# Row-limited moves of the partly filled slot tile, and the last expert's closing matmuls in another order

## The chip, the cores and the metric

The kernel runs on one core of one Trainium2 chip. The metric is device microseconds of one execution. Five engines work side by side, each in the order of its own queue: TensorE (PE in the profile, with its weight loads as PEld), VectorE (DVE), ScalarE (ACT), GpSimd (POOL) and SyncE (SP, here only issuing transfers). They meet through semaphores.

## The reference, cut to what matters

Three layers follow each other. The change touches only the third.

```python
x = attention(q, k, v, centroids)            # 2 x 8 heads, 768 rows of 64, masked by cluster
x = gelu(x @ w_in) @ w_out                   # 1536 tokens, 512 -> 2048 -> 512
logits = x @ w_gate + log1p(exp(x @ w_noise)) * noise
top2 = two largest of the 8 experts; top2_w = softmax over these two
for e in range(8):
    out[mask] += top2_w * (relu(x[mask] @ w1[e]) @ w2[e])    # 512 -> 1024 -> 512
```

## The kernel before, in words

**Slots.** Each token is written, by indirect transfers on POOL's queue, to a slot of each of its two experts in the table slot_x in memory. An expert has CAP = 448 slots: YT = 4 tiles of 128 rows, of which the fourth (index FULL = 3) has only REST = 64 rows. Before an expert runs, SP loads its slots into slot_rows (128 x 4 x 512), and TensorE turns them, so that the 512 features lie on partitions. One pass c (of DC = 4) turns 128 features: four transposes, one for each tile, into one PSUM bank. ACT and DVE then split the bank's 448 columns into a high and a low part (sx_hi, sx_lo). The fourth transpose reads all 128 rows, though only 64 were loaded. POOL's memset in line 676 has set the other 64 rows to zero once, the semaphore rest_cleared says so, and TensorE waits for it (line 1035). All transposes are in transpose mode.

**The first expert** is special. When it should start, the last 512 tokens aren't routed yet. `route_last` therefore first turns the already stored rows (`kept_slots`, eight transposes, then the small matmuls of `ranks`, then eight more), and `move_rows` adds the last tokens' rows onto the same banks with matmuls against 0/1 matrices (`moves`, built by DVE line 1602 from the result of `ranks`). Eight idle matmuls (line 831) stand ahead of the first transposes.

**The other experts.** `turn_slots(n + 1, part)` turns the rows of the next expert in the middle of expert n: part 0 (two passes, eight transposes) behind the last up-projection, part 1 behind the down-projection of piece 6. This happens for n = 0 to 6, seven times.

**The MLP of an expert** has eight pieces of 128 hidden units: `up` makes a piece (12 matmuls, each product in three parts of the fp32r type), ACT (line 1311) and DVE (line 1745) apply relu and split it (hid_done counts that), and `down` adds it to the four output banks: three matmuls for each full tile, two for the fourth tile, since its 64 columns of high and low part lie side by side. The fourth tile comes second in the order in which the last expert is closed: ORDER = (0, 3, 1, 2).

**The end.** In the last expert `down_end` does the pieces 5, 6 and 7 tile by tile. Its list of steps runs

```python
steps = [(0, last_piece - 2), (0, last_piece - 1), (1, last_piece - 2), (1, last_piece - 1),
         (0, last_piece), (1, last_piece)]
```

so that two tiles' pieces 5 and 6 come ahead of the first wait for piece 7. Meanwhile POOL gathers the rows of the other experts (line 647, got and acc; line 695, slot_rows), DVE adds them (line 1785) and SP stores the tokens. After that DVE scales the last gathers (line 1796), adds the last expert's tiles to them (`take_end`, lines 1808 and 1817), and POOL writes each tile to the output with an indirect transfer (line 703).

Of the kernel before, what the change touches and what calls it, by code (L numbers as in the profile page):

```python
# [19 lines left out]
P = 128  # L20
# [14 lines left out]
FULL = CAP // P  # L35
REST = CAP - FULL * P
YT = FULL + 1
GROUP = 256
RING = 4
# [35 lines left out]
def clustered_attention_ffn_moe(nc, q, k, v, centroids, w_in, w_out, w_gate, w_noise, noise, w1, w2, out):  # L75
    B, H, D, S = q.shape
    C = centroids.shape[1]
    DM, FF = w_in.shape
    E, _, FE = w1.shape
    N = B * S  # L80
    J = S // P
# [10 lines left out]
    GP = GROUP // P  # L92
# [28 lines left out]
    with ctx:  # L121
        def sem(name):
            return ctx.enter_context(nc.semaphore(name))

        def alloc(where, name, shape, dt):
            return where.enter_context(nc.sbuf_tensor(name, shape, dt))

        psum = ctx.enter_context(nc.psum_tensor("psum", [P, 8, 512], F32))


        ident = alloc(ctx, "ident", [P, P], F32)
# [81 lines left out]
        slot_rows = alloc(ffn, "slot_rows", [P, YT, DM], F32)  # L213
# [73 lines left out]
        group_used = sem("group_used")  # L287
        hid_ready = sem("hid_ready")
        hid_act = sem("hid_act")
        hid_done = sem("hid_done")  # L290
# [18 lines left out]
        rounds_ready = sem("rounds_ready")  # L309
        sx_in = sem("sx_in")  # L310
        slot_of_set = sem("slot_of_set")
        rest_cleared = sem("rest_cleared")
        split_hi = sem("split_hi")
        split_lo = sem("split_lo")
        moves_ready = sem("moves_ready")
# [29 lines left out]
        ORDER = (0, FULL) + tuple(range(1, FULL))  # L345

        def rows_of(j):

            return P if j < FULL else REST
# [73 lines left out]
        def turn_bank(c, first):  # L423

            return 4 + c if first else 6 + c % 2
# [155 lines left out]
        def _(pool):  # L581
# [90 lines left out]
                scatter_chunk(t)  # L672
            chain.link(nc.gpsimd.iota(slot_i[:], pattern=[[1, CAP]], base=-FAR, channel_multiplier=0))
            nc.gpsimd.tensor_copy(slot_of[:], slot_i[:]).then_inc(slot_of_set, 1)
            pool.wait_ge(slot_of_set, 1)
            nc.gpsimd.memset(slot_rows[REST:P, FULL], 0.0).then_inc(rest_cleared, 1)
            pool.wait_ge(sx_in, 2 * DMA)
            scatter_chunk(CHUNKS - 1)

            for j in range(YT):  # L680
                first = LAST_SLOT + j * P
# [57 lines left out]
        def _(pe):  # L739
            mm = nc.tensor.matmul  # L740

            def bank(n):
                return psum[:, n]
# [84 lines left out]
            def idle_rows(count, at):  # L828

                for _ in range(count):  # L830
                    mm(bank(at), ident_b[:], zeros[:].bitcast(BF16)[:, 0:CT], start=True, stop=True)
# [75 lines left out]
            def down_tile(f, slot, rest, j, pieces, held=None):  # L907

                held = f % 2 if held is None else held
                dst = bank(j)  # L910
                if rest and j == FULL:

                    both = hid_hi[:, held, j * P:]
                    mm(dst, both, down_hi[:, slot, f % GP], start=(f == 0), stop=False)
                    return mm(dst, both, down_lo[:, slot, f % GP], start=False, stop=(f == pieces - 1))  # L915
                cols = slice(j * P, (j + 1) * P)
                mm(dst, hid_hi[:, held, cols], down_hi[:, slot, f % GP], start=(f == 0), stop=False)  # L917
                mm(dst, hid_hi[:, held, cols], down_lo[:, slot, f % GP], start=False, stop=False)  # L918
                return mm(dst, hid_lo[:, held, cols], down_hi[:, slot, f % GP], start=False, stop=(f == pieces - 1))  # L919
# [11 lines left out]

            def down_end(piece0, pieces):

                last_piece = pieces - 1
                steps = [(0, last_piece - 2), (0, last_piece - 1), (1, last_piece - 2), (1, last_piece - 1),
                         (0, last_piece), (1, last_piece)]
                steps += [(i, f) for i in range(2, YT) for f in range(last_piece - 2, pieces)]
                for i, f in steps:
                    if i == 0:
                        pe.wait_ge(hid_done, piece0 + f + 1)  # L940
                    last = down_tile(f, f // GP % RING, True, ORDER[i], pieces, 2 if f == last_piece else None)
                    if i == YT - 1 and f % GP == GP - 1:
                        last.then_inc(group_used, 1)
                    elif i < YT - 1 and f == last_piece:
                        last.then_inc(y_ready, 1)

            def layer(pieces, width, rest, piece0, group0, chunk, moving_hi, moving_lo, turn, after=None,
# [23 lines left out]
            def turn_rows(f, to):  # L971

                for c in range(DC):
                    last = nc.tensor.transpose(psum[:, to, c * P:(c + 1) * P], y_sb[:, f, c * P:(c + 1) * P], ident[:])
                last.then_inc(yt_ready, 1)
# [14 lines left out]
            def ranks(p, at):  # L990

                pe.wait_ge(sel_ready, p + 1)
                for j in range(TPC):
                    dst = psum[:, at, RANK0 + j * E:RANK0 + (j + 1) * E]
                    for i in range(j):
                        mm(dst, ones_b[:], r_sel[:, i], start=(i == 0), stop=False)
                    mm(dst, before[:], r_sel[:, j], start=(j == 0), stop=True)
                for i in range(TPC):
                    last = mm(psum[:, at, RANK0 + TPC * E:RANK0 + (TPC + 1) * E], ones_b[:], r_sel[:, i],
                              start=(i == 0), stop=(i == TPC - 1))  # L1000
                last.then_inc(rank_ready, 1)

            def logits(p, j, held, at):
                if j == 0:
                    pe.wait_ge(slots_ready, LEAD + p)
                pe.wait_ge((yt_act, yt_dve)[j % 2], 2 * p + j // 2 + 1)
                for c in range(DC):
                    last = mm(psum[:, at, j * 2 * E:(j + 1) * 2 * E], yt[:, held, c * P:(c + 1) * P], wr[:, c],
                              start=(c == 0), stop=(c == DC - 1))
                if j == TPC - 1:  # L1010
                    last.then_inc(logits_ready, 1)
# [14 lines left out]
            def route_last(p):  # L1026

                pe.wait_ge(slots_ready, LEAD + p)
                for f in range(TPC):
                    pe.wait_ge((y_act, y_dve)[f % 2], LEAD + 2 * p + f // 2 + 1)  # L1030
                    turn_rows(f, 4 + f)
                for f in range(TPC):
                    logits(p, f, f, LAST)
                pe.wait_ge(sx_in, 2 * DMA)
                pe.wait_ge(rest_cleared, 1)
                idle_rows(8, FULL)
                for c in range(DC // 2):
                    kept_slots(c)
                ranks(p, LAST)
                for c in range(DC // 2, DC):  # L1040
                    kept_slots(c)
                for c in range(DC):
                    move_rows(c)

            def kept_slots(c):

                for j in range(YT):
                    mm(psum[:, turn_bank(c, True), j * P:(j + 1) * P], slot_rows[:, j, c * P:(c + 1) * P], ident[:],
                       is_transpose=True, start=(j == 0), stop=False)

            def move_rows(c):

                dst = psum[:, turn_bank(c, True), 0:CAP]
                for j in range(TPC):
                    if c == 0:
                        pe.wait_ge(split_lo, j + 1)
                        pe.wait_ge(moves_ready, j + 1)
                    mm(dst, row_hi(j)[:, c * P:(c + 1) * P], moves(j), start=False, stop=False)
                    last = mm(dst, row_lo(j)[:, c * P:(c + 1) * P], moves(j), start=False, stop=(j == TPC - 1))
                last.then_inc(sx_turned, 1)  # L1060

            route_last(CHUNKS - 1)

            PIECE0 = CHUNKS * (FF // P)

            def turn_slots(n, part, first=False):

                if part == 0:
                    pe.wait_ge(sx_in, 2 * DMA * (n + 1))
                for c in (2 * part, 2 * part + 1):  # L1070
                    if not first:
                        pe.wait_ge(sx_done, n * DC + max(c - 1, 0))
                    for j in range(YT):
                        last = nc.tensor.transpose(psum[:, turn_bank(c, first), j * P:(j + 1) * P],
                                                   slot_rows[:, j, c * P:(c + 1) * P], ident[:])
                    last.then_inc(sx_turned, 1)

            def expert_step(n, last, end=False):
                layer(FE // P, CAP, True, PIECE0 + n * (FE // P), EXPERT0 + n * EGR, CHUNKS + n,
                      lambda c: sx_hi[:, c], lambda c: sx_lo[:, c],  # L1080
                      (lambda part: None) if last else (lambda part: turn_slots(n + 1, part)),
                      turned_in=n * DC, end=end)
# [812 lines left out]
```

## Time and profile before

| | us |
|---|---|
| three runs | 921.95, 918.08, 920.74 |
| median | 920.74 |
| profiled execution, its own time | 921.95 |
| its span, first to last instruction | 920.2 |
| TensorE busy (matmuls) in the span | 897.9 |
| DVE / ACT / POOL busy | 528.1 / 420.9 / 143.6 |
| mean granted TensorE clock, share of full | 0.984 |

The profiled execution took 1.75 us more than its span. In the page a matmul's end is modelled: consecutive matmuls overlap in it, so the distance from one start to the next is what a matmul costs in a row of many, not its duration. In views that merge a run of equal instructions, x8 stands for eight of them and the second number is the time of the run.

### The profile page before, as it was taken

How to read it: one execution, taken by the hardware profiler on the slowest of the kernel's cores; microseconds unless marked ns; L12 is line 12 of the kernel's file. 1: busy time of each engine (PE TensorE's matmuls, PEld its weight loads, DVE VectorE, ACT ScalarE, POOL GpSimd, SP SyncE). 2: the span in 40 equal slices, each digit the busy share in tenths (PEclk: the TensorE clock that was granted, in tenths of full speed). 3: DMA queues.
4: the chain of work that ended last, by engine and by line, in shares of the span. 5: the costliest groups of instructions: out<-in, count | busy, mean ns of one | idle time of the engine just before them, and what ended most of it. 6: DMA issues, size and time to landing. Idle time of an engine off the chain costs nothing.

```text
span 920.2 us, 12560 instructions
## 1 busy us (share of the span) xinstructions
PE 897.9 (98%) x4353; PEld 736.0 (80%) x4355; DVE 528.1 (57%) x959; ACT 420.9 (46%) x689; POOL 143.6 (16%) x147
## 2 busy tenths in 40 slices
PE   6999999999999999999999999999999999999995
PEld 4777777777776888888888888888888888888884
DVE  6688887887866444436443645644345343434383
ACT  4577767777668222344234323424434243433420
POOL 2021221221222000002300140500000000005073
PEclk8899999999999999999999999999999999999998
DMA  5123332331353323323532343625252544527464
GB/s 125 35 70 106 94 104 67 113 109 44 97 199 134 134 99 113 116 85 120 169 123 91 125 150 130 222 95 197 95 186 89 190 146 145 170 92 268 164 195 164
DMA packets 84302, 119.00 MB, mean 129 GB/s; under 512 B 19258, under 2 KB 47930, under 8 KB 84256
## 3 DMA queue, kind: packets, MB, share of 16 engines
q1 hardware_dynamic: 79328, 104.08, 35.1%
q0 software_dynamic: 4928, 14.35, 4.5%
q8 instruction: 24, 0.39, 0.2%
q14 instruction: 22, 0.18, 0.1%
HBM read 89.12 MB, written 29.39 MB: 129 GB/s over the span
## 4 chain that ended last, share of the span: by engine, by line
PE 78%; DVE 9%; issue 5%; POOL 4%; DMA 1%; ACT 1%; SPq 1%; POOLq 0%; DVEq 0%; ACTq 0%
PE psum L818 10%; PE psum L902 9%; PE psum L904 9%; PE psum L903 9%; PE psum L917 8%; PE psum L919 8%; PE psum L918 8%; PE psum L783 3%; PE psum L803 3%; PE psum L804 3%; DVE neg_max L1432 2%; POOL got L647 2%; POOL acc L647 1%; DVE recip L1456 1%; PE psum L915 1%
## 5 line engine op out<-in xcount | busy, mean ns | idle before, releaser
L818 PE MATMUL psum<-probs,vx 128*128 128x386 f32 x384 | 156.4, 489 | 0.4 <-ACT probs L1141 0.4
L917 PE MATMUL psum<-down_hi,hid_hi 128*128 128x512 f32 x384 | 151.1, 393 | 0.7 <-DVE hid_lo L1704 0.7
L919 PE MATMUL psum<-down_hi,hid_lo 128*128 128x512 f32 x384 | 149.9, 390 | 0.0
L918 PE MATMUL psum<-down_lo,hid_hi 128*128 128x512 f32 x384 | 149.9, 390 | 0.0
L1311 ACT ACTIVATE hid_hi<-psum 128x448 fp32r<-128x448 f32 x64 | 35.0, 546 | 180.4 <-PE psum L904 180.4
L1141 ACT ACTIVATE probs<-psum 128x384 f32<-128x384 f32 x192 | 90.5, 489 | 55.9 <-PE psum L804 53.3
L1432 DVE TENSOR_REDUCE neg_max<-psum 128x1 f32<-128x768 f32 x96 | 91.3, 955 | 25.8 <-PE psum L783 22.2
L1745 DVE SCALAR_TENSOR_TENSOR hid_lo<-psum,hid_hi 128x384 fp32r<-128x384 f32 x64 | 35.6, 556 | 117.4 <-ACT hid_hi L1311 117.4
L1284 ACT ACTIVATE gelu<-psum 128x512 f32<-128x512 f32 x48 | 28.7, 598 | 157.2 <-PE psum L904 157.2
L803 PE MATMUL psum<-qa,ka 102*128 102x384 f32 x192 | 93.9, 489 | 0.6 <-DVEq L1445 0.5
L903 PE MATMUL psum<-sx_lo,up_hi 128*128 128x448 f32 x256 | 93.5, 365 | 0.0
L902 PE MATMUL psum<-sx_hi,up_hi 128*128 128x448 f32 x256 | 93.5, 365 | 0.0
L904 PE MATMUL psum<-sx_hi,up_lo 128*128 128x448 f32 x256 | 93.5, 365 | 0.0
L1467 DVE TENSOR_TENSOR up_lo<-raw,up_hi 128x1024 fp32r<-128x1024 f32 x56 | 68.5, 1222 | 38.6 <-ACT down_hi L1176 38.5
L919 PEld LDWEIGHTS psum<-down_hi,hid_lo 128*128 128x128 f32 x384 | 72.0, 188 | 15.5
L917 PEld LDWEIGHTS psum<-down_hi,hid_hi 128*128 128x128 f32 x384 | 72.1, 188 | 14.7 <-issue 1.1
L918 PEld LDWEIGHTS psum<-down_lo,hid_hi 128*128 128x128 f32 x384 | 72.2, 188 | 13.9
L1703 DVE CAST hid_hi<-gelu 128x512 fp32r<-128x512 f32 x48 | 20.8, 432 | 106.5 <-ACT gelu L1284 106.5
L902 PE MATMUL psum<-xt_hi,up_hi 128*128 (+1 forms) x192 | 76.3, 398 | 0.0
L904 PE MATMUL psum<-xt_hi,up_lo 128*128 (+1 forms) x192 | 74.9, 390 | 0.0
L903 PE MATMUL psum<-xt_lo,up_hi 128*128 (+1 forms) x192 | 74.8, 389 | 0.0
L618 POOL TENSOR_TENSOR off<-less_sum,near 64x384 f32<-64x384 f32 x32 | 39.8, 1245 | 216.7 <-ACT near L1156 216.7
(208 smaller groups left out, 1548.1 us busy)
## 6 DMA issues: line engine op xcount, KB each, us to landing
raw<-in_moe_w SPq DMA_DIRECT2D x64, 512.0 KB, 4.2
raw<-in_moe_w_in SPq DMA_DIRECT2D x24, 512.0 KB, 3.5
raw<-in_moe_w_out SPq DMA_DIRECT2D x24, 512.0 KB, 5.1
slot_x<-zeros SPq DMA_DIRECT2D x7, 1024.0 KB, 5.6
slot_rows<-slot_x SPq DMA_DIRECT2D x8, 768.0 KB, 6.7
raw_q<-in_q SPq DMA_DIRECT2D x30, 192.0 KB, 3.3
raw_k<-in_k SPq DMA_DIRECT2D x30, 192.0 KB, 3.7
slot_y<-y_sb SPq DMA_DIRECT2D x7, 768.0 KB, 3.6
```

Source lines behind the costliest of these rows:

```text
L618: nc.gpsimd.tensor_tensor(off[rows], less_sum[rows], near[rows], ALU.mult).then_inc(off_ready, 1)
L803: mm(dst, ka[0:ROWS, n % SLOTS, keys], qa[0:ROWS, n % SLOTS, queries], start=True, stop=False)
L818: mm(psum[:, 5 + half, 0:WIDE], vx[:, n % 2, c], probs[:, at % SLOTS], start=(c == 0), stop=(c == J - 1)).then_inc(unit_done, 1)
L902: mm(dst, up_hi[:, slot, c, cols], moving_hi(c), start=(c == 0), stop=False)
L903: mm(dst, up_hi[:, slot, c, cols], moving_lo(c), start=False, stop=False)
L904: last = mm(dst, up_lo[:, slot, c, cols], moving_hi(c), start=False, stop=(c == DC - 1))
L917: mm(dst, hid_hi[:, held, cols], down_hi[:, slot, f % GP], start=(f == 0), stop=False)
L918: mm(dst, hid_hi[:, held, cols], down_lo[:, slot, f % GP], start=False, stop=False)
L919: return mm(dst, hid_lo[:, held, cols], down_hi[:, slot, f % GP], start=False, stop=(f == pieces - 1))
L1141: copy(probs[:, at % SLOTS, 0:HALF], psum[:, 2 + at % SLOTS, 0:HALF], ACT.Exp, scale=float(D) ** -0.5)\
L1432: dv.tensor_reduce(neg_max[:, m % 2, i:i + 1], psum[:, held:held + 2, 0:HALF], AX.XY, ALU.max, negate=True)\
L1467: dv.tensor_tensor(up_lo[:, slot], raw1[:, stage], up_hi[:, slot].bitcast(F32), ALU.subtract)
```

## The change

It does three things.

1. The fourth tile's transposes take only its 64 loaded rows, against a 64 x 64 identity, and write 64 columns. The memset, its semaphore and TensorE's wait are gone.
2. `kept_slots` no longer sets transpose mode: its 16 products are ordinary fp32 matmuls against the identity.
3. `down_end` closes one tile after another: all of pieces 5, 6, 7 of tile 0, then of the fourth tile, then of tiles 1 and 2.

```diff
-            pool.wait_ge(slot_of_set, 1)
-            nc.gpsimd.memset(slot_rows[REST:P, FULL], 0.0).then_inc(rest_cleared, 1)
...
-                last_piece = pieces - 1
-                steps = [(0, last_piece - 2), (0, last_piece - 1), (1, last_piece - 2), (1, last_piece - 1),
-                         (0, last_piece), (1, last_piece)]
-                steps += [(i, f) for i in range(2, YT) for f in range(last_piece - 2, pieces)]
-                for i, f in steps:
+                for i, j in enumerate(ORDER):
+                    for f in range(pieces - 3, pieces):
...
-                pe.wait_ge(rest_cleared, 1)
...
-                    mm(psum[:, turn_bank(c, True), j * P:(j + 1) * P], slot_rows[:, j, c * P:(c + 1) * P], ident[:],
-                       is_transpose=True, start=(j == 0), stop=False)
+                    rows = rows_of(j)
+                    mm(psum[:, turn_bank(c, True), j * P:j * P + rows], slot_rows[0:rows, j, c * P:(c + 1) * P],
+                       ident[0:rows, 0:rows], start=(j == 0), stop=False)
...
-                        last = nc.tensor.transpose(psum[:, turn_bank(c, first), j * P:(j + 1) * P],
-                                                   slot_rows[:, j, c * P:(c + 1) * P], ident[:])
+                        rows = P if j < FULL else REST
+                        last = nc.tensor.transpose(psum[:, turn_bank(c, first), j * P:j * P + rows],
+                                                   slot_rows[0:rows, j, c * P:(c + 1) * P], ident[0:rows, 0:rows])
```

On TensorE, at the rows of the first expert, this stood before (a row is a matmul, what it writes, what it reads, the size of the output; L1048 is `kept_slots`, L831 the idle matmuls, L996 to L999 `ranks`):

```order
L831 MATMUL psum<-zeros,ident_b 128x512 x8
L1048 MATMUL psum<-ident,slot_rows 128x128 x8
L997 MATMUL psum<-r_sel,before 128x8
```

And this stands there now (L1042 is `kept_slots`):

```order
L828 MATMUL psum<-zeros,ident_b 128x512 x8
L1042 MATMUL psum<-ident,slot_rows 128x128 x3
L1042 MATMUL psum<-ident,slot_rows 128x64
L1042 MATMUL psum<-ident,slot_rows 128x128 x3
L1042 MATMUL psum<-ident,slot_rows 128x64
L991 MATMUL psum<-r_sel,before 128x8
```

Nothing moved; every fourth product of the eight has become half as wide. The same holds for the eight behind `ranks` and for the 16 of each `turn_slots`.

On TensorE, at the end of the last expert, this stood in `down_end` before (L917 to L919 are the three matmuls of a full tile, L914 and L915 the two of the fourth tile; "waits" names the semaphore):

```order
L917 MATMUL psum<-down_hi,hid_hi 128x512 [waits hid_done]
L918 MATMUL psum<-down_lo,hid_hi 128x512
L919 MATMUL psum<-down_hi,hid_lo 128x512
L914 MATMUL psum<-down_hi,hid_hi 128x512
L915 MATMUL psum<-down_lo,hid_hi 128x512
L914 MATMUL psum<-down_hi,hid_hi 128x512
L915 MATMUL psum<-down_lo,hid_hi 128x512
L917 MATMUL psum<-down_hi,hid_hi 128x512 [waits hid_done]
```

The first of these rows begins piece 6 of tile 0, the last one begins piece 7. Now (L914 to L916 are the matmuls of a full tile, L911 and L912 those of the fourth):

```order
L914 MATMUL psum<-down_hi,hid_hi 128x512 [waits hid_done]
L915 MATMUL psum<-down_lo,hid_hi 128x512
L916 MATMUL psum<-down_hi,hid_lo 128x512
L914 MATMUL psum<-down_hi,hid_hi 128x512 [waits hid_done]
L915 MATMUL psum<-down_lo,hid_hi 128x512
L916 MATMUL psum<-down_hi,hid_lo 128x512
L911 MATMUL psum<-down_hi,hid_hi 128x512
L912 MATMUL psum<-down_lo,hid_hi 128x512
```

The wait for piece 7 stands directly behind piece 6 of the same tile; four matmuls of the fourth tile that stood ahead of it now stand behind it.

## Rows read from the trace of the kernel before

**Rows 1.** Page, parts 1 and 4: engines' busy time; chain that ended last.

```profile
PE 897.9 (98%) x4353; PEld 736.0 (80%) x4355; DVE 528.1 (57%) x959; ACT 420.9 (46%) x689; POOL 143.6 (16%) x147
...
PE 78%; DVE 9%; issue 5%; POOL 4%; DMA 1%; ACT 1%; SPq 1%; POOLq 0%; DVEq 0%; ACTq 0%
```

**Rows 2.** Groups of PE, 584 to 614 us: line, shapes, count, busy, mean, idle.

```profile
L904 PE MATMUL psum<-sx_hi,up_lo 128*128 128x448 f32 x25 | 9.1, 365 | 0.0
```

**Rows 3.** Chain in order of time, around the first expert's rows: start, us, what.

```profile
564.01 3.59 PE psum L1008 x32
...
570.90 0.87 PE psum L1048 x8
572.20 0.93 PE psum L1048 x8
```

**Rows 4.** Timeline of the same place: start, us, engine, line, output and inputs.

```profile
571.44 0.19 DVE L1635 TENSOR_TENSOR r_sel<-r_one 128x32 bf16<-128x32 f32 x1
...
571.69 0.10 PEld L997 LDWEIGHTS psum<-r_sel,before 128*128 128x128 bf16 x1 [0.15 <-DVE r_sel L1635]
...
572.54 1.54 DVE L1602 TENSOR_SCALAR xt_hi<-slot_of,key 128x448 fp32r<-128x448 f32 x4
```

**Rows 5.** Windows there: busy by engine (PE first), then granted clock, DMA, GB/s.

```profile
567.40:570.40 3.00, 2.78 (x8) 1.07 (x10) 1.59 (x15) 0.66 (x3) 0.00 (x0) 0.50 0.00 0
570.40:572.00 1.60, 1.60 (x22) 1.32 (x21) 1.10 (x9) 0.21 (x1) 0.00 (x0) 0.92 0.00 0
```

**Rows 6.** Three lines' weight loads: count, shortest/median/longest in ns, array size.

```profile
L1074 PEld LDWEIGHTS psum<-ident,slot_rows x112: 138/140/143, 614.0 to 866.5; 128*128 128x128 f32 x112
L791 PEld LDWEIGHTS psum<-ident,neg_max x16: 84/84/128, 25.5 to 271.7; 128*6 128x6 f32 x16
L1008 PEld LDWEIGHTS psum<-wr,yt x96: 187/192/293, 384.6 to 567.2; 128*128 128x128 f32 x96
```

**Rows 7.** Timeline of PE in an attention head, around a transpose on six array columns.

```profile
42.91 0.27 PE L791 MATMUL psum<-ident,neg_max 128*6 128x128 f32 x1
...
42.94 0.42 PE L803 MATMUL psum<-qa,ka 102*128 102x384 f32 x1
...
43.20 0.34 PE L804 MATMUL psum<-qb,kb 128*128 128x384 f32 x1
...
43.38 0.49 PE L818 MATMUL psum<-probs,vx 128*128 128x386 f32 x1
```

**Rows 8.** Chain, one of the runs of transposes in the expert loop.

```profile
614.37 0.87 PE psum L1074 x8
```

**Rows 9.** Timeline of the last expert's end: PE and DVE.

```profile
903.07 0.22 DVE L1745 SCALAR_TENSOR_TENSOR hid_hi<-psum,hid_hi 128x64 fp32r<-128x64 f32 x1
...
903.59 0.39 PE L917 MATMUL psum<-down_hi,hid_hi 128*128 128x512 f32 x1
...
908.57 0.39 PE L919 MATMUL psum<-down_hi,hid_lo 128*128 128x512 f32 x1
```

**Rows 10.** Timeline of the last 15 us: DVE and POOL.

```profile
905.31 1.67 DVE L1796 TENSOR_SCALAR slot_rows<-slot_rows,end_meta 128x512 f32<-128x512 f32 x4 [2.03 <-DMA slot_rows<-slot_y,end_low]
...
908.68 1.45 POOL L703 DMA_INDIRECT out<-y_sb,end_row  x1 [7.99 <-DVE y_sb L1808]
909.12 1.40 DVE L1808 SCALAR_TENSOR_TENSOR y_sb<-psum,end_meta,slot_rows 128x512 f32<-128x512 f32 x2
...
911.69 0.99 POOL L703 DMA_INDIRECT out<-y_sb,end_row  x1 [0.30 <-issue]
```

**Rows 11.** Chain from 840 us on: first and longest of POOL's 12 gathers (got).

```profile
875.59 2.04 POOL got L647
...
879.43 3.44 POOL got L647
```

**Rows 12.** Timeline of POOL: the memset, and the transfers behind it.

```profile
546.82 0.68 POOL L676 MEMSET slot_rows<- 64x512 f32 x1
...
577.40 1.00 POOL L642 DMA_INDIRECT slot_x<-y_sb,slot_now  x1 [29.89 <-DVEq L1656]
```

More of the change, by code:

```diff
@@ L311, in clustered_attention_ffn_moe @@
         slot_of_set = sem("slot_of_set")
-        rest_cleared = sem("rest_cleared")
         split_hi = sem("split_hi")
@@ L932, in down_end @@
             def down_end(piece0, pieces):
-                last_piece = pieces - 1
-                steps = [(0, last_piece - 2), (0, last_piece - 1), (1, last_piece - 2), (1, last_piece - 1),
-                         (0, last_piece), (1, last_piece)]
-                steps += [(i, f) for i in range(2, YT) for f in range(last_piece - 2, pieces)]
-                for i, f in steps:
[L939 to L944, printed above, removed]
+                for i, j in enumerate(ORDER):
+                    for f in range(pieces - 3, pieces):
+                        if i == 0:
+                            pe.wait_ge(hid_done, piece0 + f + 1)
+                        last = down_tile(f, f // GP % RING, True, j, pieces, 2 if f == pieces - 1 else None)
+                        if i == YT - 1 and f % GP == GP - 1:
+                            last.then_inc(group_used, 1)
+                    if i < YT - 1:
                         last.then_inc(y_ready, 1)
```

## The prediction, made before the changed kernel ran

> **What bounds the kernel now.** I read the page's engine table and its chain first. TensorE is busy in 98% of the span, and it is 78% of the chain that ended last [rows 1]. Second, I asked for the groups of TensorE's instructions inside the expert loop, to see whether it waits there: the last column, idle time, is 0.0 [rows 2]. Until the seventh expert's results are stored, a microsecond more or less on TensorE is therefore one more or less at the end. Third, I followed the chain in order of time. From 875.59 us on, when the seventh expert's rows are stored and POOL's gathers of them begin [rows 11], it no longer runs through TensorE, but through these gathers, a landing, DVE and POOL's output transfers. In these last 45 us a delay of TensorE counts only if it outlasts POOL's chain. All three parts of the change are read against these two regions: full price up to the end of the seventh expert, slack behind it.
>
> **Part 1a: 28 narrower transposes in the expert loop.** A run of eight full transposes takes 0.87 us, 0.109 us each [rows 8]; there are 14 such runs in seven experts (112 transposes), and in each two of the eight become 64 wide: 28 in all. What is the floor of a narrow one? Half the columns at the same rate are 0.109 / 2 = 0.055 us. The load of its weights stays 128 columns wide. A load of six columns is recorded with 84 ns and one of 128 columns in transpose mode with 140 ns, so the load itself is some 56 ns, or 59 for all 128 columns [rows 6]. It runs beside the stream before it, or eight could not fit in 0.87 us. I take 0.06 us, since both limits are there. The gain is 28 x (0.109 - 0.06) = 1.4 us. The bounds are 0 (load and overhead, not columns, set the 0.109) and 1.5 (half of everything).
>
> A rule of the Trainium skill stands against that load time: its page "TensorE: Matmul & The Clock Gate", section "LDWEIGHTS (loading the stationary operand)", gives the columns divided by 1.2 as the nanoseconds, which makes 107 ns for 128 columns. By it this gain would be about zero and the sum 1.4 us higher; the trace's 56 ns between a six-column and a full load doesn't agree with it for transposes.
>
> **Part 1b: the memset and its wait.** The memset takes 0.68 us at 546.8, and POOL's next transfer starts at 577.4 after 29.9 us of waiting [rows 12]. TensorE passed the wait for it long after it was done. Price 0, hidden by that waiting.
>
> **Part 2: kept_slots as ordinary fp32 matmuls.** Such a product is recorded as two matmuls, each with its own load. The nearest row is the routing product, also fp32: its 16 products are 32 records in 3.59 us, 0.112 us each, with only 16 columns moving, so their loads set that pace [rows 3]; the load is recorded with 192 ns against a transpose's 140 [rows 6]. With 128 columns moving the stream is about as long as a transpose's, 0.109 us, so load and stream are nearly equal. Overlapped, as they are in a transpose, a record costs 0.112; one behind the other, 0.22. I take 0.112, because the transposes show the overlap. The narrow ones gain nothing here, as the load sets the pace. So 16 products cost 32 x 0.112 = 3.6 us in place of 0.87 + 0.93 = 1.8 [rows 3]: plus 1.8 us, with bounds of plus 1.7 and plus 5.2.
>
> Is any of it hidden? The first eight end just as r_sel, which `ranks` needs, is ready: the load for it waits only 0.15 us [rows 4]. So the first half delays `ranks` by nearly its full 0.9 us. DVE's building of the move matrices follows `ranks` and is delayed by the same 0.9 us, but the second half is 0.9 us longer too. TensorE needed the first matrix behind the second half, at 572.20 + 0.93 = 573.13 [rows 3], when the first of DVE's four (0.39 us each from 572.54 on) was just done [rows 4]; now it needs it 1.8 us later and gets it 0.9 us later. Both halves count in full. The clock is at its lower level, 1.2 GHz, for the idle matmuls and returns to 2.4 GHz at about 570.5, as the first transposes begin [rows 5]. If its return fell one such stretch later, these products would cost up to 3.6 us more.
>
> **Part 3: down_end.** Before, piece 7 of tile 0 begins at 903.59, 22 matmuls ahead of the last one at 908.57 (0.226 us each), and DVE's last instruction for that piece ends at 903.07 + 0.22 = 903.29 [rows 9]. In the new order four of these matmuls no longer stand ahead of it, so TensorE would be ready at 903.59 - 0.91 = 902.68 and has to wait to about 903.3: some 0.6 us of stall, and its last matmul, at 908.57 before, starts 0.6 us later. Who needs it? The DVE step for the last two tiles begins at 909.12; its second half, at 909.8, needs the last bank, which would be there at 908.57 + 0.39 + 0.6 = 909.6. The tiles before wait longer: the first one is ready before DVE has finished scaling the gathers, at 905.31 + 1.67 = 906.98. Behind DVE comes POOL, which starts the third output at 911.69 and the fourth 1.3 us later, while DVE ends at 910.52: 2.4 us of slack [rows 10]. Price 0, covered by POOL's output transfers; without that cover it is plus 0.6.
>
> **Sum.** -1.4 + 0 + 1.8 + 0 = +0.4 us. The profiled execution would go from 921.95 to 922.3 and its span from 920.2 to 920.6. It was the slowest of three runs; against their median, 920.74, the sum is 921.1.
>
> **The rivals.**
>
> *The array has to empty when the number of its rows in use changes.* No matmul of the kernel before uses 64 rows or fewer: 80 and 102 are the smallest. Now 32 narrow products (28 and 4) stand between full ones, each with a change before and one behind, 64 in all. If each makes TensorE wait until the array is empty, the price is what a lone transpose takes beyond its stream: 0.27 - 0.11 = 0.16 us [rows 7]. That is 64 x 0.16 = 10.2 us, and the time 931.3. It decides the sign from 0.066 us a change on (4.2 us over the sum). Against it speaks a neighbour: a transpose on six array columns, L791, stands between full matmuls. The 384 columns of L804 take 43.38 - 43.20 = 0.18 us, so L803, as wide, began at about 43.02, 0.11 us after L791, which is L791's own stream [rows 7]. Changing the columns in use costs nothing visible, but no row shows a change of rows. The Trainium skill, page "TensorEngine Tiling (Array Packing)", section "Key Properties", says just this: changing the tiling mode drains TensorE, and its modes include 64 x 128. For the columns the trace does not agree with it.
>
> *Narrow transposes cost as much as full ones.* The 0.109 us is then not the columns'. Only the plus 1.8 us is left: 922.5.
>
> *POOL's gathers run more freely.* One of the 12 gathers takes 3.44 us where most take about 1 us [rows 11], and it coincides with DVE instructions on the weights. It lies on the chain's last part. A small shift of the phases may remove it: -2.4 us, 918.7. It may as well bring another one.
>
> *The change does nothing that counts:* the fp32 products are as quick as the transposes, and the gain stands: 919.3, the fast end.
>
> **How the numbers follow.** Sum as forecast 0.48; narrow transposes at full price 0.17; the array empties 0.22; freer gathers 0.07; the fast end 0.06. The likeliest time is 921.1. Three runs of one kernel spread over 3.9 us, so about 2 us either side are the measurement's. At the lower end 919.3 and 918.7 are taken in, with little below 918.0. At the upper end 922.5, a serial load in part 2 (921.1 + 3.4 = 924.5) and a change of rows that costs a third of its bound (924.5) are taken in: 926.5. What is left out, most of the emptying array and a little below, is about 2 in 10. A measurement of this kernel can tell about 0.5%, 4.6 us, from no change. Only the emptying array passes that on the slow side, nearly always: with a little for a serial load that meets the lower clock, 0.20 slower. Nothing found reaches 4.6 us on the fast side: 0.03. The rest, 0.77, is within.
>
> **What would show it.** In the expert loop a run of eight transposes should take 0.77 us, not 0.87; 0.87 would mean the second rival, and 1.4 or more the emptying array, with gaps around every fourth. In `kept_slots` 32 records at 0.112 us, and the first move matmul 1.8 us later against the idle matmuls. In `down_end` a wait for DVE line 1745's result of 0.6 us, and POOL's four output transfers at an unchanged distance from the seventh expert's last store. The prediction would be wrong if the changes of rows cost over 0.066 us each, or if the last output transfer waited for TensorE's last bank.

## The result, and the profile after

The changed kernel takes 929.0 us in the median of four runs (928.13 to 930.17); the kernel before takes 919.52 us beside it. The ratio is 1.0101, with a 95% interval of 1.0073 to 1.0131: slower by 1%, some 9.3 us. The prediction said 921.1, with 926.5 as its upper end.

The page of the changed kernel, parts 1 and 4 (against [rows 1]):

```profile
PE 911.4 (97%) x4371; PEld 741.2 (79%) x4371; DVE 529.7 (57%) x959; ACT 423.5 (45%) x689; POOL 140.4 (15%) x146
...
PE 85%; DVE 10%; issue 2%; ACT 1%; another core or an unknown queue 1%; DMA 0%; POOL 0%; POOLq 0%; DVEq 0%; ACTq 0%; SPq 0%
```

TensorE has 18 more matmul records (16 of them are the halves of the fp32 products; a few records can be missing from a trace) and 13.5 us more busy time. The profiled execution itself took 937.3 us, 8 us more than the kernel's other runs: ACT stood for 4.1 us near 588 us and for 7.3 us near 866 us without a cause that the profile shows (it names only a source outside the core's known queues), the second of them in the line below, from the table of waits between 850 and 875 us. No other profile of this study has such a wait. Its cause stays open, so I leave it out of the account and read stretches, not the span.

```profile
ACT hid_hi L1306 <- remote: 7.3, 1, 7.3
```

The chain around the first expert's rows (start, us, what; L1002 is the routing product, L828 the idle matmuls, L1042 `kept_slots`), against [rows 3]:

```profile
564.83 3.48 PE psum L1002 x32
568.31 3.24 PE psum L828 x8
571.55 2.43 PE psum L1042 x16
574.43 2.36 PE psum L1042 x16
```

The two halves of `kept_slots` take 4.79 us in place of 1.80: plus 3.0, where 1.8 was forecast. Further down, the same chain has the runs of eight transposes of two consecutive experts (L1069 is the line of `turn_slots`), against [rows 8]:

```profile
622.26 1.21 PE psum L1069 x8
626.19 1.21 PE psum L1069 x8
664.64 1.21 PE psum L1069 x8
668.58 1.21 PE psum L1069 x8
```

A run takes 1.21 us, not 0.87 and not the 0.77 of the forecast. From expert to expert it is 664.64 - 622.26 = 42.38 us. Before it was 41.36: of the kernel before, the chain has

```profile
655.73 0.87 PE psum L1074 x8
```

for the next expert, and 655.73 - 614.37 [rows 8] = 41.36. So an expert's step is 1.02 us longer, and seven make 7.1. With the 3.0 us of the first expert's rows that is 10.1 us; 9.3 were measured, and the difference of 0.8 is within the interval. Where the time goes is seen in the groups of TensorE's loads and matmuls by shape (count, busy us, mean ns, idle before):

```profile
L1069 PEld LDWEIGHTS psum<-ident,slot_rows 128*128 128x128 f32 x84 | 9.8, 140 | 2.4
L1069 PE MATMUL psum<-ident,slot_rows 64*128 64x64 f32 x28 | 7.6, 272 | 0.0
L1069 PEld LDWEIGHTS psum<-ident,slot_rows 64*128 64x128 f32 x28 | 3.8, 136 | 4.7 <-issue 4.7
```

The narrow load itself is short (136 ns), but in front of each of the 28 the load row stands empty for 0.17 us (4.7 in total), with nothing named that it waited for. And the narrow matmuls are recorded with 272 ns, where the full ones have 281 here and 272 in the kernel before. This is the shape of the rival that the array empties when the rows in use change. The forecast of what the profile would show for it, 1.4 us or more a run, was a little high.

The end of this execution differs too: its chain runs through TensorE to the last bank (PE 85%, POOL 0%, where [rows 1] had 78% and 4%). TensorE's load for piece 7, DVE's step for the last tile and POOL's last output transfer:

```profile
920.34 0.19 PEld L914 LDWEIGHTS psum<-down_hi,hid_hi 128*128 128x128 f32 x1 [1.34 <-DVE hid_hi L1740]
...
926.78 0.75 DVE L1803 SCALAR_TENSOR_TENSOR y_sb<-psum,end_meta,slot_rows 128x512 f32<-128x512 f32 x1 [1.29 <-PE psum L916]
...
928.33 0.98 POOL L700 DMA_INDIRECT out<-y_sb,end_row  x1 [0.96 <-DVE y_sb L1803]
```

TensorE waits 1.34 us for piece 7, DVE 1.29 us for the last bank, and the last output transfer stands idle 0.96 us, against 0.30 between two transfers that wait for nothing: 0.66 us of it is the wait for DVE's step on the last bank. That is the second of the two signs that the prediction named for being wrong. This is the execution in which ACT had stood twice, so how often it happens in the others isn't shown.

### The profile page after: what moved, and what is told of

It reads as the page before. It is cut to its first block, busy times and chain, and to the rows that moved or that the text cites. A ratio compares the mean times of both kernels' runs of the same rounds, so it can differ in the third digit from the quotient of the medians.

```text
span 935.5 us, 12592 instructions
## 1 busy us (share of the span) xinstructions
PE 911.4 (97%) x4371; PEld 741.2 (79%) x4371; DVE 529.7 (57%) x959; ACT 423.5 (45%) x689; POOL 140.4 (15%) x146
## 4 chain that ended last, share of the span: by engine, by line
PE 85%; DVE 10%; issue 2%; ACT 1%; another core or an unknown queue 1%; DMA 0%; POOL 0%; POOLq 0%; DVEq 0%; ACTq 0%; SPq 0%
PE psum L901 10%; PE psum L899 10%; PE psum L914 10%; PE psum L900 10%; PE psum L915 9%; PE psum L916 9%; PE psum L815 9%; PE psum L780 3%; PE psum L800 3%; DVE neg_max L1427 3%; PE psum L801 2%; PE psum L1069 2%; PE psum L912 2%; PE psum L911 2%; PE psum L757 1%
## 5 line engine op out<-in xcount | busy, mean ns | idle before, releaser
L914 PE MATMUL psum<-down_hi,hid_hi 128*128 128x512 f32 x384 | 151.8, 395 | 6.6 <-DVE hid_hi L1740 5.9
L916 PE MATMUL psum<-down_hi,hid_lo 128*128 128x512 f32 x384 | 149.8, 390 | 0.0
L915 PE MATMUL psum<-down_lo,hid_hi 128*128 128x512 f32 x384 | 149.8, 390 | 0.0
L914 PEld LDWEIGHTS psum<-down_hi,hid_hi 128*128 128x128 f32 x384 | 72.1, 188 | 23.1 <-DVE hid_hi L1740 7.6
L916 PEld LDWEIGHTS psum<-down_hi,hid_lo 128*128 128x128 f32 x384 | 72.1, 188 | 15.4
L915 PEld LDWEIGHTS psum<-down_lo,hid_hi 128*128 128x128 f32 x384 | 72.1, 188 | 13.7
```

## The experiments

Two theories stood against each other at first. **A**: each change between 128 and 64 rows in use stalls TensorE. **B**: the first expert's longer start makes other engines late, and the rest follows. The first four kernels do one part of the change alone. Where a cut of code leaves lines out, "..." stands for them.

**Narrow transposes in the expert loop alone.**

```diff
-                        last = nc.tensor.transpose(psum[:, turn_bank(c, first), j * P:(j + 1) * P],
-                                                   slot_rows[:, j, c * P:(c + 1) * P], ident[:])
+                        rows = P if j < FULL else REST
+                        last = nc.tensor.transpose(psum[:, turn_bank(c, first), j * P:j * P + rows],
+                                                   slot_rows[0:rows, j, c * P:(c + 1) * P], ident[0:rows, 0:rows])
```

> The kernel before, with only the fourth tile's transposes of turn_slots (28 in seven experts) cut to 64 rows and 64 columns. Theory A (each change between 128 rows and 64 rows in use stalls TensorE): in the profile of the changed kernel a run of eight with two narrow ones, with the matmul behind it, takes 0.53 us more than before; 14 such runs make plus 7.4 us, ratio 1.008. Theory B (the narrow transposes cost nothing extra and the 9 us come from the first expert's fp32 products and what waits behind them): minus 1.4 us to 0, ratio 0.999.

Measured: 929.48 us against 921.28 of the kernel before beside it, ratio 1.0096 (1.0063 to 1.0129). These 28 narrow transposes alone carry about the whole loss of time. Its chain shows the same runs, and the first expert's rows as before:

```profile
569.67 0.87 PE psum L1048 x8
570.98 0.93 PE psum L1048 x8
...
613.15 1.21 PE psum L1075 x8
...
655.54 1.21 PE psum L1075 x8
```

Theory B isn't needed for the loss, and its own range (minus 1.4 us to 0) is excluded: nothing about the first expert's start differs here. The step from expert to expert is 42.39 us, 1.03 more than before.

**kept_slots as fp32 matmuls, all full.**

```diff
-                       is_transpose=True, start=(j == 0), stop=False)
+                       start=(j == 0), stop=False)
```

> The kernel before, with only transpose mode taken off the 16 products of kept_slots; they stay 128 rows and 128 columns. Theory A: 32 records of 0.112 us in place of 16 of 0.11: plus 1.8 us, ratio 1.002, and nothing behind it. Theory B (the delay makes DVE and ACT late for the first expert, so TensorE waits there too): plus 4 to 8 us.

Measured: 921.29 against 921.28 us, ratio 1.001 (0.9989 to 1.003). The chain has

```profile
571.31 1.85 PE psum L1048 x16
573.49 1.89 PE psum L1048 x16
```

so 32 records take 3.74 us, 0.117 each, and the two halves cost 1.9 us more than before. Load and stream do overlap. The stretch is measured well; the whole kernel's interval holds both plus 1.9 us (0.2%) and nothing. Its upper end is plus 2.8 us, so it excludes theory B's plus 4 to 8.

**The new order of down_end alone.**

```diff
-                for i, f in steps:
...
+                for i, j in enumerate(ORDER):
+                    for f in range(pieces - 3, pieces):
...
```

> The kernel before, with only the new order of down_end. As predicted: TensorE waits 0.6 us for piece 7 and its last matmul is 0.6 us later against the last up-projection, but the end does not move: ratio 1.000. The rival: the end moves with it, plus 0.6 us or more, ratio 1.001.

Measured: 920.93 against 921.28 us, ratio 1.0 (0.9976 to 1.0024). The timeline of the end (DVE's last instruction for piece 7, TensorE's load and matmul that begin piece 7, then DVE's step for the last tile and POOL's last output transfer), against [rows 9, 10]:

```profile
902.39 0.21 DVE L1742 SCALAR_TENSOR_TENSOR hid_hi<-psum,hid_hi 128x64 fp32r<-128x64 f32 x1
902.66 0.19 PEld L917 LDWEIGHTS psum<-down_hi,hid_hi 128*128 128x128 f32 x1 [0.55 <-DVE hid_hi L1742]
902.66 0.51 PE L917 MATMUL psum<-down_hi,hid_hi 128*128 128x512 f32 x1
...
909.11 0.75 DVE L1805 SCALAR_TENSOR_TENSOR y_sb<-psum,end_meta,slot_rows 128x512 f32<-128x512 f32 x1 [0.63 <-PE psum L919]
...
911.61 0.98 POOL L703 DMA_INDIRECT out<-y_sb,end_row  x1 [0.30 <-issue]
```

TensorE's load waits 0.55 us for piece 7, as forecast. The cover holds in this execution, but one link was thinner than I had put it: DVE's last step waits 0.63 us for the last bank. It still ends at 909.86, and POOL, which does one output transfer after another, starts the last one at 911.61. The interval of the whole times, 2.2 us to either side, can't tell the forecast from the rival's 0.6 us; the timeline decides, for one execution.

The forecast's 2.4 us of slack varies from execution to execution. From the end of DVE's last step to the start of the last transfer it is 1.75 us here, between 1.2 and 2.5 in the kernels with the old order, and 0.9 in the kernel with the new order and 72 rows below. The hand-over from DVE to POOL is still in it: 0.8 us in the changed kernel, where POOL did wait for it.

**Narrow products in kept_slots alone, in transpose mode.**

```diff
+                    rows = rows_of(j)
+                    mm(psum[:, turn_bank(c, True), j * P:j * P + rows], slot_rows[0:rows, j, c * P:(c + 1) * P],
+                       ident[0:rows, 0:rows], is_transpose=True, start=(j == 0), stop=False)
```

> The kernel before, with only the fourth tile's products of kept_slots cut to 64 rows and 64 columns, in transpose mode as before. Theory A: four narrow ones at plus 0.26 us each, 1.0 us on the two groups of eight, ratio 1.001. Theory B (row changes cost nothing): minus 0.2 us.

Measured: 921.98 against 921.28 us, ratio 1.0007 (0.9989 to 1.0025). One half of its `kept_slots` in the chain:

```profile
570.98 1.36 PE psum L1049 x8
```

That is 0.43 us more than the second half before [rows 3], 0.21 for each of its two narrow products, and the timeline has the 0.17 us of empty load row ahead of each. So the price is tied neither to the expert loop nor to the ordinary fp32 products of the changed `kept_slots`. The whole kernel's interval can't resolve 1 us.

The next four ask what the price is paid for.

**72 rows in place of 64.** The narrow transposes of the expert loop take 72 rows and 72 columns, eight of the rows zero.

```diff
+                        rows = P if j < FULL else 72
...
```

> The kernel before, with the fourth tile's transposes of turn_slots cut to 72 rows and 72 columns (the memset stays, since rows 64 to 71 are read). Theory A (the stall belongs to 64 rows, another setting of the array than 128, and 72 still runs in the setting of 128): no stall; 28 transposes of 0.06 in place of 0.109 us, minus 1.2 us, a run of eight in 0.78 us, ratio 0.999. Theory C (any transpose on fewer rows or columns than its neighbours stalls, or a narrow one is slow in itself): plus 7 us, a run of eight in 1.2 us, ratio 1.008.

Measured: 918.85 against 919.83 us, ratio 1.0 (0.9985 to 1.0016), which excludes theory C. The groups and the chain:

```profile
L1075 PE MATMUL psum<-ident,slot_rows 72*128 72x72 f32 x28 | 6.4, 228 | 0.0
L1075 PEld LDWEIGHTS psum<-ident,slot_rows 72*128 72x128 f32 x28 | 3.9, 139 | 0.0
```

```profile
613.38 0.79 PE psum L1075 x8
...
654.65 0.79 PE psum L1075 x8
```

There is no empty load row, a run takes 0.79 us, and a narrow matmul is recorded with 228 ns against 270 of a full one. Eight rows more, and the stall is gone, so it isn't that rows are left out. This kernel moves 72 columns where the other moved 64, but few moving columns alone don't bring the stall: in the kernel before, the routing product with 16 moving columns follows 16 full transposes without an empty load row (the second line starts 1.75 us behind the first, 16 x 0.109).

```profile
562.10 1.91 PE L974 MATMUL psum<-ident,y_sb 128*128 128x128 f32 x16
...
563.85 3.75 PE L1008 MATMUL psum<-wr,yt 128*128 128x16 f32 x32
```

So the stall belongs to the 64 rows. Other numbers of rows over 64 don't pay either. In an attention head of the kernel before, matmuls of 384 columns on 80, 102 and 128 rows follow each other in steps of 0.18 us, their stream alone:

```profile
46.73 0.34 PE L783 MATMUL psum<-ka,qa 80*128 80x384 f32 x1
46.91 0.34 PE L803 MATMUL psum<-qa,ka 102*128 102x384 f32 x1
47.09 0.34 PE L804 MATMUL psum<-qb,kb 128*128 128x384 f32 x1
```

The step between experts of the kernel with 72 rows is 41.27 us, 0.09 less than before, so of the 0.08 us that each of the two runs gains about half is lost again in the matmuls behind it.

**The same 28 narrow transposes in 14 pairs.** Here they have 64 rows again; the second pass of each part begins with its narrow tile. Both passes wait for the later one's condition, ahead of the first.

```diff
...
+                for j in range(YT):
+                    last = turn(c0, j)
...
+                for j in (FULL,) + tuple(range(FULL)):
+                    last = turn(c1, j)
```

> The kernel with narrow transposes of 64 rows in turn_slots alone, but the second pass of each part does its narrow tile first, so that the two narrow ones stand side by side: the same 28, with half the changes. Theory A (the price is paid at a change): 14 pairs at 0.31 us of stall, less 28 x 0.055 us saved: plus 2.8 us, ratio 1.003. Theory D (each narrow transpose is slow whatever stands beside it): plus 7.1 us, ratio 1.008.

Measured: 922.92 against 919.83 us, ratio 1.003 (1.0014 to 1.0046), as theory A had it. The line of the transposes, its loads and the idle time ahead of them:

```profile
L1074 PEld LDWEIGHTS psum<-ident,slot_rows x112: 134/139/143, 615.2 to 870.3; 128*128 128x128 f32 x84, 64*128 64x128 f32 x28
...
  issue: 2.3, 14
```

28 narrow transposes, but 14 waits: only the first of a pair has one. A run takes 1.07 us. The price is that of a change, not of a narrow transpose.

**Each narrow transpose done twice, apart.**

```diff
-                    for j in range(YT):
+                    for j in (0, FULL) + tuple(range(1, YT)):
+                        rows = P if j < FULL else REST
...
```

> The kernel with narrow transposes of 64 rows in turn_slots alone, and each of them done twice, once behind tile 0 and once at its own place (the second writes the same values again): 56 narrow ones, each alone among full ones. Theory A: 56 x 0.363 us in place of 28 x 0.109 us, plus 17.3 us, ratio 1.019. If the stall were a wait for something else that comes once in a pass (the slots' load, DVE's sx_done), the second would cost its 0.06 us only: plus 9 us, ratio 1.010.

Measured: 936.87 against 919.83 us, ratio 1.0188 (1.0165 to 1.0211). Theory A had 1.019. The chain:

```profile
613.29 1.92 PE psum L1075 x10
...
657.14 1.92 PE psum L1075 x10
```

A pass with two narrow ones pays twice, so no wait that comes once in a pass is behind it. The step between experts is 43.85 us, 2.49 more than before, for eight narrow transposes where four full ones stood. With a narrow one at 0.086 us (an estimate from 72 rows: the step fell by 0.09 us for four narrow ones, so 0.109 less 0.023) and a stall S for each: 8 x 0.086 - 4 x 0.109 + 8 x S = 2.49 gives S = 0.28. The kernel with 28 gives 4 x (0.086 - 0.109 + S) = 1.03, which is 0.28 as well.

**The whole change with 72 rows for 64.** fp32 `kept_slots`, new `down_end`, memset back.

```diff
-                    rows = rows_of(j)
+                    rows = P if j < FULL else 72
...
-                        rows = P if j < FULL else REST
+                        rows = P if j < FULL else 72
```

> The changed kernel with one thing altered: wherever it takes 64 rows of the fourth tile it takes 72 (which needs the memset back). kept_slots is fp32, down_end in the new order. Theory A: the whole loss of 9 us goes; left are plus 2.2 us of the fp32 products and minus 1.2 us of the narrow ones: plus 1.0 us against the kernel before, ratio 1.001. If the loss had another source in the changed kernel, ratio 1.008 or more.

Measured: 920.59 against 919.83 us, ratio 1.001 (0.9994 to 1.0027). The loss of the changed kernel is gone with the 64 rows alone. What stays, 0.8 us, has an interval that holds both the forecast's plus 0.4 and zero. The two halves of its `kept_slots` take 3.79 us, where the changed kernel has 4.79:

```profile
569.42 1.95 PE psum L1046 x16
571.70 1.84 PE psum L1046 x16
```

**Best version that the experiments point to:** transpose mode and 72 rows in both places.

> The kernel before, with the fourth tile cut to 72 rows and columns both in turn_slots and in kept_slots, everything in transpose mode, the memset kept: the saving without the stall. Theory A: 28 + 4 narrow transposes at 0.06 us in place of 0.109: minus 1.5 us, ratio 0.998. If TensorE's saved time is taken back elsewhere (POOL's gathers, the first expert's wait for the split rows): ratio 1.000.

Measured: 919.42 against 920.34 us, ratio 0.9992 (0.9979 to 1.0005). The sign is as expected, but the interval holds zero: no version is shown to beat the kernel before.

## Why the prediction was wrong

**The bound: right; the path at the end: only in part.** TensorE sets the time up to the seventh expert's end. The 1.03 us by which each expert's step grew appear in the total (7.2 us of some 8.2). Behind that point the profiles differ: in the kernel with `down_end` alone the end didn't wait for TensorE, in the profile of the changed kernel it did, by 0.66 us.

**Part 1a, the narrow transposes: the step that failed.** It priced a narrow transpose by its own stream and load, and took the gain of 28 x 0.05 us. That description fits 72 rows: 0.79 us a run, though half of the gain is taken back by what follows, so minus 0.6 us and not minus 1.4. For 64 rows a stall of 0.28 us stands beside it, which the sum had put at nothing, and 28 of them turn the term from -1.4 into +7.1 us.

**The rival that was right, and its weight.** "The array has to empty when the number of its rows in use changes" was priced at 2 x 0.16 = 0.32 us for each narrow transpose. 0.28 was measured, 0.14 for each change and so over the 0.066 named as a sign of being wrong, and its 931.3 us compares with 929.0. The runs show the stall, what brings it and its size; that the array empties in it is argued from the size alone. It got a chance of 0.22, because the neighbour in the trace, a transpose on six columns, paid nothing for its change [rows 7]. That row is right and says nothing about 64 rows: the inference from a change of columns to a change of rows was the error. Nor is it so that no row shows a change of rows: in [rows 7] itself L803 uses 102 rows and L804 behind it 128, at no cost. What no row showed was a change to 64. The Trainium skill's page "TensorEngine Tiling (Array Packing)", section "Key Properties", says that changing the tiling mode drains TensorE, and makes no such difference. For the change from 128 to 64 rows the traces here agree with it, by 0.28 us a pair of changes, and they narrow it: 72 and 102 rows pay nothing beside 128, nor 80 beside 102.

**The load time of the Trainium skill.** The rule of 107 ns for the load of 128 columns (page "TensorE: Matmul & The Clock Gate", section "LDWEIGHTS (loading the stationary operand)") would have kept narrow transposes at full price. The trace with 72 rows does not agree: a run of eight takes 0.79 in place of 0.87 us, so the loads don't set that pace.

**Part 1b: nothing speaks against it.** No run takes out the memset alone. In the changed kernel, without it, POOL's next transfer still stood waiting for 32.2 us, against 29.9 with it [rows 12], so the 0.68 us were hidden there as forecast.

**Part 2, the fp32 products: the mechanism right.** 1.9 us alone against 1.8 forecast. In the changed kernel it is 3.0, since its four narrow ones pay the stall as well: the remaining 1.05 us (4.79 - 3.74) are 0.26 for each, and with 72 rows for 64 they are gone (3.79).

**Part 3, down_end: the wait right, the cover too thick.** Alone it has 0.55 us of wait against 0.6 and an end that doesn't wait for it. The slack of 2.4 us behind DVE was read from one execution, with the hand-over to POOL in it; in the profile of the changed kernel, disturbed as it is, it was used up. At 0.66 us this is not what moved the time out of the range.

**Freer gathers: seen as well.** Up to the start of the next transfers, the 12 gathers take 18.15 us in the changed kernel's profile and 19.88 in the profile before. The last output transfer starts 36.3 us after the first gather in place of 37.4, so in this profile some 1.1 us went against the loss. The forecast had priced this rival at minus 2.4 us.

**What the range missed.** A stall for each narrow transpose has two plausible sizes, none or about 0.3 us, and little in between. A range that ended at a third of the rival's bound covered the unlikely middle and left out the second size.

## What to carry to other kernels

Count how often consecutive matmuls change between 128 rows in use and 64; here each narrow one among full ones cost 0.28 us, more than twice a whole 128-column transpose, so padding a 64-row tile to a few rows more, or to all 128, is cheaper than cutting it. (Fewer than 64 rows weren't measured, nor 65 to 71.) If 64 rows are needed, put those matmuls side by side, so that the change is paid once. And a slack should be read from more than one execution, without the hand-over in it. Where a rival's price is large and the only evidence against it is from another kind of case, the range should reach its price.

## What the runs showed of the hardware that was not expected

- TensorE stalls between matmuls on 128 and on 64 rows (0.28 us for the way there and back), not between 128 and 72 rows. Of this, 0.17 us are seen as an empty load row ahead of the narrow load. How the rest divides between the way there and the way back wasn't separated.
- TensorE's clock around the first expert's rows differs between executions of nearly the same kernel. In [rows 5] it is at its lower level, 1.2 GHz, during the idle matmuls. In the kernel with narrow products in `kept_slots` it stayed at 2.4 GHz there, TensorE then waited 1.1 us for r_sel, and it fell when the move matmuls came (windows: busy by engine, PE first, then the granted clock, DMA share, GB/s):

```profile
569.50:572.20 2.70, 1.73 (x22) 1.28 (x22) 1.93 (x12) 0.18 (x1) 0.00 (x0) 0.96 0.00 0
572.20:575.30 3.10, 3.10 (x9) 2.73 (x9) 2.46 (x16) 0.00 (x0) 0.00 (x0) 0.50 0.03 5
```

A low stretch that falls on the idle matmuls costs little, and one that falls on the 448-column move matmuls costs about half of its 3.1 us: they start 0.37 us apart there and 0.20 us apart at 2.4 GHz. That may be part of the spread of some 4 us between runs of one kernel; it wasn't tested.
